# Attention and two routed expert layers on one core: code moved at both ends of the attention

## The chip, the cores and the metric

The kernel runs on one core of one Trainium2 chip. Its five instruction queues are PE (TensorE, matmuls and transposes; PEld is its weight load), DVE (VectorE), ACT (ScalarE), POOL (GpSimd) and SP (SyncE, which here only issues DMAs). The metric is the device time of one execution in microseconds (us).

## What is computed

```python
# q, k, v: (4 batches, 8 heads, 768, 64) f32; n_global = 8, n_local = 96
scores = q @ k.T / 8 - slope[h] * dist        # per batch and head
scores = where(global key or 0 <= row - col < n_local, scores, -1e9)
a = softmax(scores);  x = (a @ v) as (3072 tokens, 512)

# first expert layer: each token to the expert of its largest logit
e = argmax(x @ w_gate);  g = softmax(x @ w_gate)[e] * sigmoid(x @ w_output_gate)[e]
y = g * (relu(x @ w1[e]) @ w2[e])             # 8 experts, 512 -> 1024 -> 512
# second expert layer: greedy assignment with 384 tokens per expert
out = relu(y @ v1[e2]) @ v2[e2]
```

## The kernel before

**Attention.** 32 heads are worked as 16 pairs of heads, two pairs in each round (`two_pairs(it, ...)`): round 0 is written out, rounds 1 to 6 are a loop, and the last (`LAST`, 7) is written out again. A round has six steps t, each for two row tiles s of 128 queries. With these inputs only a band of 256 keys is needed for a row tile, and the kernel has a function for that form on each engine (`pe_banded`, `dve_banded`, `act_banded`, `pool_banded`) and one for the general form (`..._dense`). `by_form` chooses at run time: it reads a flag, and each engine goes into an If that holds its banded function or into the Else that holds its dense one. The Else stands behind the If in the instruction stream, and what comes after both stands behind the Else.

In a step, PE computes scores (`score`, L478), turns a tile of q and k of a later pair (`turn`, L461, bank `ps_t`), turns the output columns of two steps earlier (`turn_back`, L518), turns the probabilities (`turn_probs`, L491) and multiplies by v (`value`, L509, bank `ps_o[:, 0]`). DVE adds the bias (L688), makes the low parts of q and k (`low_qk`, L662 to L670; q and k are held as a high and a low part, and scores take three products), copies turned probabilities (L699) and divides by the sums (`norm`, L717). ACT does the exponentials (L820), the high parts (`high_qk`, L798 to L804), the other half of the copies (L829), and copies the output columns from PSUM to `o_cols` (`copy_cols`, L836). The bias table is made once on DVE (`dve_far`, L561 to L592), ahead of the low parts of pair 0. `turn` of a pair waits for its loads (`qk_in`); from pair 1 on it also waits until the low parts have been read out of `ps_t` (`qk_kept`).

**Loads and stores.** SP issues, in this order: pairs 0 and 1 of k, q and v, the gate weights, a 2 MB broadcast of the second gate, then q and k of pair 2. After that, for each pair in turn: q and k of the pair after the next but one once `qk_turned` allows it, v two pairs ahead once `valued` allows it, and the six stores of x once `normed` allows them. The first weights (`raw`, L2108) are issued behind the last stores.

**Logits and routing.** Behind the If and Else, `pe_logits` waits for all norms, turns the 24 tiles of x (L943, four banks in rotation), and multiplies each group of two tiles by the gates (`group_logits`, L970); ACT and DVE make high and low parts (L985, L1004), and in the last eight tiles also the first expert's w1 (L990, L1011). `dve_routing1` is one chain of small operations that sorts the tokens into blocks; PE helps with ranks (L1061) and a table (`pe_table`, L1075). From the table DVE makes the row numbers (`rows_i`, L1167), POOL copies one column of them (L1557) and gathers the first block's 128 rows of x (L1560) into `xg`. ACT meanwhile converts w2 and `wg_all` (L1228, L1231), then makes an exponential that the gates need (L1234).

**First block.** `keep_busy(18)` gives PE 18 matmuls of 512 columns on zeros (L1067), whose result nobody reads; then come `turn_x(0)` (L1261), `up(0)` (L1275), `turn_x(1)`, a second table (L1075), `turn_h(0)` (L1286), and from there blocks of 24 plus 24 matmuls (L1275, L1298) in a loop. DVE's part of that start is `low_x(0)`, the gate table, the low part of w2, `low_x(1)`, and then `dve_gates` (L1213), which waits for PE's second table.

## Time and profile before

| | us |
|---|---|
| median of 3 runs | 1052.54 |
| lowest and highest | 1049.64, 1052.82 |
| the profiled execution | 1050.72 |
| its span in the trace | 1049.0 |
| attention (first work to last norm) | 0 to 213 |
| logits, routing, start of the first block | 213 to 283 |
| blocks of the first expert layer | 283 to 632 |
| end of that layer, second routing, second layer | 632 to 1049 |

The profile gives each instruction's start and duration from the span's start, and for an engine's idle time what ended it. "issue" stands for idle time that ended with nothing the profile shows. PEclk is the clock granted to TensorE as a share of 2.4 GHz; it has two levels, 1.00 and 0.50, and values between them are averages over a stretch. Times in the rows below are of the profiled execution.

### The profile page before, as it was taken

Reading aid. Unit: us, or ns where it says so; the run is one execution under the profiler, and the core shown is the slowest. Engines: PE = TensorE matmul, PEld = TensorE weight load, DVE = VectorE, ACT = ScalarE, POOL = GpSimd, SP = SyncE. Lnnn points to the kernel's source line nnn. Section 1 sums busy time; section 2 is a strip of 40 time slices with the busy share of each in tenths; the row PEclk is TensorE's granted clock in tenths of the full one; section 3 lists DMA queues with packets and bytes.
Section 4 is the critical chain, followed back from the end, with each engine's and each line's share of the span. In section 5 each row is a group of like instructions: output and inputs, shape, how many; then the busy total and the mean of one; then the engine's idle time right before and its main releaser. Section 6 shows DMA issues by size and latency. Waiting matters only on the chain.

```text
span 1049.0 us, 22340 instructions
## 1 busy us (share of the span) xinstructions
PE 919.3 (88%) x6394; PEld 773.8 (74%) x6397; DVE 680.0 (65%) x1823; ACT 451.2 (43%) x982; POOL 191.1 (18%) x247
## 2 busy tenths in 40 slices
PE   6889999884999999999999985444599999999994
PEld 4767777773788888888888873333398989899993
DVE  4778888758766968869877784555554645463521
ACT  3778888746344352535525350000042524343410
POOL 1222322300111111111111110000203212321211
PEclk8899999987899999999999996555699999999998
DMA  9577677342351524515334251000135353635100
GB/s 213 110 160 169 161 172 165 85 178 81 111 201 41 209 69 171 200 50 200 121 129 150 93 190 57 2 2 2 34 108 209 123 198 133 220 115 203 42 31 31
DMA packets 146567, 129.40 MB, mean 123 GB/s; under 512 B 102464, under 2 KB 114752, under 8 KB 146368
## 3 DMA queue, kind: packets, MB, share of 16 engines
q1 hardware_dynamic: 137696, 99.68, 31.8%
q0 software_dynamic: 8800, 28.84, 8.1%
q8 instruction: 35, 0.57, 0.2%
q14 instruction: 36, 0.29, 0.1%
HBM read 107.79 MB, written 20.71 MB: 122 GB/s over the span
## 4 chain that ended last, share of the span: by engine, by line
PE 72%; DVE 9%; issue 6%; SPq 5%; DMA 3%; DVEq 2%; ACT 1%; POOL 0%; ACTq 0%; POOLq 0%
PE ps_o L1298 14%; PE ps_s L1275 14%; PE ps_o L1640 9%; PE ps_s L1624 6%; PE ps_pT L1624 6%; PE ps_s L1640 4%; PE ps_t L1801 3%; DMA qn<-in_q 2%; PE ps_pT L1286 2%; PE ps_o L509 2%; SPq L2053 2%; SPq L2072 1%; PE ps_t L461 1%; PE ps_t L1261 1%; PE ps_s L478 1%
## 5 line engine op out<-in xcount | busy, mean ns | idle before, releaser
L1298 PE MATMUL ps_o<-w_split_parts,hs 128*128 x696 | 169.2, 399 | 6.3 <-issue 6.3
L1275 PE MATMUL ps_s<-w_split_parts,xs 128*128 x696 | 165.8, 394 | 1.1 <-ACT xs L1367 1.1
L1298 PEld LDWEIGHTS ps_o<-w_split_parts,hs 128*128 128x128 f32 x696 | 130.1, 190 | 33.9 <-issue 7.1
L1485 DVE SCALAR_TENSOR_TENSOR product<-y_sb,wg_all 128x512 bf16<-128x512 f32 x224 | 145.8, 689 | 11.4 <-issue 6.7
L1275 PEld LDWEIGHTS ps_s<-w_split_parts,xs 128*128 128x128 f32 x696 | 128.9, 189 | 26.6 <-issue 1.3
L820 ACT ACTIVATE arena_p<-arena_p,min_s 128x256 f32<-128x256 f32 (+1 forms) x192 | 92.3, 484 | 29.6 <-DVE min_s L688 28.8
L1640 PE MATMUL ps_o<-w_split_parts,hs 128*128 128x512 f32 x384 | 94.1, 397 | 0.0
L1476 DVE TENSOR_TENSOR w_split_parts<-raw,w_split_parts 128x1024 f32 (+1 forms) x68 | 78.7, 1221 | 20.3 <-ACT w_split_parts L1386 19.0
L1640 PEld LDWEIGHTS ps_o<-w_split_parts,hs 128*128 128x128 f32 x384 | 70.2, 188 | 15.9 <-ACT hs L1674 2.9
L1720 DVE TENSOR_TENSOR w_split_parts<-raw,w_split_parts 128x1024 fp32r<-128x1024 f32 x56 | 68.6, 1225 | 18.7 <-ACT w_split_parts L1682 18.5
L1375 ACT ACTIVATE hs<-ps_pT 128x512 fp32r<-128x512 f32 x58 | 31.7, 597 | 113.1 <-PE ps_pT L1286 113.1
L1667 ACT ACTIVATE xs<-ps_t 128x512 fp32r<-128x512 f32 x22 | 13.2, 599 | 142.0 <-PE ps_t L1611 141.8
L1624 PE MATMUL ps_s<-xs,w_split_parts 128*128 128x384 f32 x384 | 69.6, 335 | 1.5 <-issue 1.5
L688 DVE CUSTOM_DVE_ANT_0 arena_p<-ps_s,arena_b 128x256 f32<-128x256 f32 (+1 forms) x144 | 54.1, 398 | 24.0 <-PE ps_o L478 8.2
L1624 PEld LDWEIGHTS ps_s<-xs,w_split_parts 128*128 128x128 f32 x384 | 67.3, 188 | 2.8 <-issue 1.7
L1624 PE MATMUL ps_pT<-xs,w_split_parts 128*128 128x384 f32 x384 | 69.1, 334 | 0.0
L1624 PEld LDWEIGHTS ps_pT<-xs,w_split_parts 128*128 128x128 f32 x384 | 66.8, 188 | 0.0
L1674 ACT ACTIVATE hs<-ps_s 128x384 fp32r<-128x384 f32 x32 | 15.8, 493 | 117.9 <-PE ps_s L1624 117.9
L1386 ACT ACTIVATE w_split_parts<-raw 128x1024 f32 (+1 forms) x64 | 62.4, 1055 | 9.0 <-issue 7.3
L1710 DVE SCALAR_TENSOR_TENSOR hs<-ps_s,hs 128x384 fp32r<-128x384 f32 x32 | 17.7, 553 | 75.0 <-ACT hs L1674 75.0
L1682 ACT ACTIVATE w_split_parts<-raw 128x1024 fp32r<-128x1024 f32 x56 | 59.0, 1054 | 0.0
L1566 POOL DMA_DIRECT2D y_rows<-y_sb x31 | 17.9, 577 | 211.3 <-ACT y_sb L1393 206.4
(307 smaller groups left out, 1690.5 us busy)
## 6 DMA issues: line engine op xcount, KB each, us to landing
raw<-in_moe_w SPq DMA_DIRECT2D x32, 2048.0 KB, 9.2
y_rows<-y_sb POOLq DMA_DIRECT2D x31, 256.0 KB, 2.3
kn<-in_k SPq DMA_DIRECT2D x32, 192.0 KB, 3.5
qn<-in_q SPq DMA_DIRECT2D x32, 192.0 KB, 3.6
vn<-in_v SPq DMA_DIRECT2D x32, 192.0 KB, 2.9
x_rows<-arena_x SPq DMA_DIRECT2D x96, 64.0 KB, 1.6
va<-in_v SPq DMA_DIRECT2D x32, 120.0 KB, 2.7
wg_rows<-in_moe_w_gate SPq DMA_DIRECT2D x1, 2048.0 KB, 7.6
```

The costliest lines, as they stand in the source:

```text
L688: nc.vector.tensor_tensor_reduce(out=neg_b[:, s % STEPS_HELD, hh, 0:w], in0=SCORE_BANKS[t % 2 * 2 + hh][:, side:side + w], in1=bias[:, par ...
L820: nc.scalar.activation(probs_b[:, s % STEPS_HELD, hh, 0:w], neg_b[:, s % STEPS_HELD, hh, 0:w], ACT.Exp, scale=-1.0, bias=min_s[:, slot:slo ...
L1275: last = nc.tensor.matmul(ps_s[:, f, :], xs[:, a, c * P:(c + 1) * P], weights(par, w, cols), start=(n == 0), stop=(n == len(passes) - 1))
L1298: last = nc.tensor.matmul(ps_o[:, 0, :], hs[:, a, c * P:(c + 1) * P], weights(par, 2 + w, slice(c * DM, (c + 1) * DM)), start=(n == 0), st ...
L1375: nc.scalar.activation(hs[:, 0, f * HALF:(f + 1) * HALF], ps_pT[:, f, :], ACT.Copy).then_inc(h_high, 1)
L1386: nc.scalar.activation(weights(par, 2 * kind, cols), raw[:, kind, cols], ACT.Copy).then_inc(hi_done, 1)
L1476: low = nc.vector.tensor_tensor(weights(par, 2 * kind + 1, cols), raw[:, kind, cols], as_f32(weights(par, 2 * kind, cols)), ALU.subtract)
L1485: nc.vector.scalar_tensor_tensor(product[:, e % 2, :], y_sb[:], 1.0, wg_all[:, e, :], ALU.mult, ALU.mult, accum_out=log_now[:, e:e + 1])
L1624: last = nc.tensor.matmul(HID_BANKS[f % 4], ws[:, par, w, at:at + P], xs2[:, a, c, :], start=(n == 0), stop=(n == len(passes) - 1))
L1640: last = nc.tensor.matmul(OUT_BANKS[j], hs2[:, a, c, j * P:(j + 1) * P], ws[:, par, 2 + w, f * DM:(f + 1) * DM], start=(half == 0 and n == ...
L1682: nc.scalar.activation(ws[:, 1 - par, 2 * kind, cols], raw[:, kind, cols], ACT.Copy).then_inc(hi_done, 1)
L1720: low = nc.vector.tensor_tensor(ws[:, 1 - par, 2 * kind + 1, cols], raw[:, kind, cols], as_f32(ws[:, 1 - par, 2 * kind, cols]), ALU.subtract)
```

## The change

Six edits. (1) On DVE, the low parts of pair 0 come ahead of the last part of the bias table (`low_parts()` in `dve_far`). (2) PE has ten matmuls on the constant tile `warm` (result unread) between the turns of pair 0 and `score(0, 0)`. (3) Pair 1's second turn goes to the bank `ps_o[:, 0]` and stands next to its first. (4) In the last round, `value` of step 5 writes the bank `ps_s[:, 0]` and stands ahead of `turn_back` of step 4; `o_cols` has two halves; `value` waits once for both tiles' probabilities. (5) Logits and routing, and DVE's start of the experts, go inside both branches of `by_form`; in the banded branch the first three tiles wait for the first batch's norms alone, the fourth for all, and the rotation of banks is another. ACT's last exponential (`act_gates`) and everything after it stay behind the branches; `keep_busy` has 10 instead of 18. (6) The first gather takes its row numbers from `rows_i` itself, without POOL's copy.

```diff
--- before
+++ after
@@ -138,8 +138,8 @@
 arena_p = at("arena_p", starts[6], [P, 3 * PART_P])
-o_cols = at("o_cols", 4 * sum(sizes), [P, 2 * P])
-assert 4 * (sum(sizes) + 2 * P) <= WSPLIT // 2
+o_cols = at("o_cols", 4 * sum(sizes), [P, 2, 2 * P])
+assert 4 * (sum(sizes) + 4 * P) <= WSPLIT // 2
@@ -419,16 +419,23 @@
     two_pairs(LAST, True)
+ps_t_whole = ps_t[:]
...
-    return FIRST_TURNS[g] if isinstance(pair, int) and pair == 0 else ps_t[:]
+    if isinstance(pair, int) and (pair == 0 or pair == 1 and g == 1):
+        return FIRST_TURNS[g]
+    return ps_t_whole
...
+def out_bank(it, t):
+
+    return ps_s[:, 0, :] if isinstance(it, int) and it == LAST and t == TWOS - 1 else ps_o[:, 0, :]
@@ -440,7 +447,7 @@
             for nth, g in turns_of(first, last_one).get(t, [])[which]]
-FRONT, MORE = slice(0, 1), slice(1, None)
+FRONT, MORE = slice(0, 2), slice(2, None)
@@ -453,7 +460,7 @@
             pe.wait_ge(qk_in[par], nth * 64 + 64)
-        if not (isinstance(pair, int) and pair == 0):
+        if turn_bank(pair, g) is not FIRST_TURNS[g]:
@@ -497,16 +504,15 @@
             pe.wait_ge(v_in[par], it * 96 + 96)
-        pe.wait_ge(normed, it * 6 + t + NORM0)
+        pe.wait_ge(normed, it * 6 + t - (isinstance(it, int) and it == LAST and t == TWOS - 1) + NORM0)
+        pe.wait_ge(p_kept, it * 12 + 2 * t + 2 + ATT0)
                 for s in (2 * t, 2 * t + 1):
-
-            pe.wait_ge(p_kept, it * 12 + s + 1 + ATT0)
...
-                    last = nc.tensor.matmul(ps_o[hh * D:hh * D + D, 0, at:at + P], tiles[:, par, a:a + D],
+                    last = nc.tensor.matmul(out_bank(it, t)[hh * D:hh * D + D, at:at + P], tiles[:, par, a:a + D],
@@ -515,7 +521,7 @@
         for j in range(2):
-            last = nc.tensor.transpose(ps_o[:, 0, j * P:(j + 1) * P], o_cols[:, j * P:(j + 1) * P], ident[:])
+            last = nc.tensor.transpose(out_bank(it, t)[:, j * P:(j + 1) * P], o_cols[:, t % 2, j * P:(j + 1) * P], ident[:])
@@ -536,12 +542,14 @@
         if last_one:
+            value(it, TWOS - 1)
                     turn_back(it, TWOS - 2)
-            value(it, TWOS - 1)
...
+    for n in range(10):
+        nc.tensor.matmul(ps_pT[:, 1, :], warm[:, 0:P], warm, start=True, stop=True)
@@ -584,6 +592,7 @@
     global_far(tmp[:, P:2 * P], key[:, 0:P], tmp[:, 0:P])
+    low_parts()
@@ -711,7 +719,7 @@
         dve.wait_ge(o_turned, it * 6 + t + 1)
-        o3 = ps_o[:, 0, 0:2 * P].rearrange("p (i c) -> p i c", c=D)
+        o3 = out_bank(it, t)[:, 0:2 * P].rearrange("p (i c) -> p i c", c=D)
@@ -736,8 +744,11 @@
                 norm(it, t)
-    for g in range(3):
-        low_qk(0, 0, g)
+    def first_low():
+        for g in range(3):
+            low_qk(0, 0, g)
+
+    dve_far(dve, True, first_low)
@@ -830,10 +841,10 @@
         act.wait_ge(valued, it * 24 + 4 * t + 4 + ATT0)
-        if not (isinstance(it, int) and it == 0 and t == 0):
-
-            act.wait_ge(o_turned, it * 6 + t)
-        nc.scalar.activation(o_cols[:], ps_o[:, 0, 0:2 * P], ACT.Copy).then_inc(o_copied, 1)
+        if not (isinstance(it, int) and it == 0 and t < 2):
+
+            act.wait_ge(o_turned, it * 6 + t - 1)
+        nc.scalar.activation(o_cols[:, t % 2, :], out_bank(it, t)[:, 0:2 * P], ACT.Copy).then_inc(o_copied, 1)
@@ -905,14 +916,16 @@
     pool_attention(pool, False)
-def by_form(eng, banded, dense):
+def by_form(eng, banded, dense, then):
...
+        then(eng, True)
             with eng.Else():
                 dense(eng)
+        then(eng, False)
@@ -922,7 +935,7 @@
-TURN_BANKS = [ps_t[:], ps_o[:, 0, :], ps_o[:, 1, :], ps_s[:, 2, :]]
+TURN_BANKS = [ps_t[:], ps_o[:, 1, :], ps_s[:, 2, :], ps_o[:, 0, :]]
@@ -931,11 +944,15 @@
     return TURN_BANKS[t % 4].rearrange("p (c r) -> p c r", c=DC)
-def pe_logits(pe):
-
-    pe.wait_ge(normed, 3 * PAIRS + NORM0)
+def pe_logits(pe, ahead):
+
+    if not ahead:
+        pe.wait_ge(normed, 3 * PAIRS + NORM0)
             pe.wait_ge(consts, 8)
             for t in range(TILES):
+        if ahead and t in (0, 3):
+
+            pe.wait_ge(normed, (3 * HP if t == 0 else 3 * PAIRS) + NORM0)
@@ -1230,8 +1247,10 @@
     nc.scalar.activation(wg_all[:], wg_rows[:].rearrange("p d e -> p e d"), ACT.Copy).then_inc(wg_all_made, 1)
+def act_gates(act):
+
             act.wait_ge(r_s, 2)
-    nc.scalar.activation(m_open[:, 0:C], t2b[:, 0:C], ACT.Exp, scale=-1.0).then_inc(r_e, 1)
+    nc.scalar.activation(m_open[:, 0:TILES], t2b[:, 0:TILES], ACT.Exp, scale=-1.0).then_inc(r_e, 1)
@@ -1531,13 +1553,15 @@
             last_block(b)
-    nc.vector.memset(logits_2[:], 0.0)
-    dve.drain()
-    dve.wait_ge(wg_all_made, 1)
-    low_x(0)
-    dve_gate_table(dve)
-    low_w(0, 0, 1, range(4), n=0)
-    low_x(1)
+    if start_only:
+        nc.vector.memset(logits_2[:], 0.0)
+        dve.drain()
+        dve.wait_ge(wg_all_made, 1)
+        low_x(0)
+        dve_gate_table(dve)
+        low_w(0, 0, 1, range(4), n=0)
+        low_x(1)
+        return
@@ -1550,15 +1574,17 @@
     def gather(b):
+        rows = rows_i
...
-        nc.gpsimd.tensor_copy(row_now[:], rows_i[:, bass.ds(b, 1)]).then_inc(row_copied, 1)
-        pool.wait_ge(row_copied, b + 1)
-        apart(pool)
+            rows = row_now
+            nc.gpsimd.tensor_copy(row_now[:], rows_i[:, bass.ds(b, 1)]).then_inc(row_copied, 1)
+            pool.wait_ge(row_copied, b)
+            apart(pool)
                 nc.gpsimd.indirect_dma_start(out=xg[:], out_offset=None, in_=x_dram[:, :],
-                                     in_offset=bass.IndirectOffsetOnAxis(row_now[:, 0:1], 0),
+                                     in_offset=bass.IndirectOffsetOnAxis(rows[:, 0:1], 0),
@@ -2175,6 +2201,11 @@
     pool_experts2(pool)
+def dve_first_route(dve, is_banded):
+    dve_logits(dve)
+    dve_routing1(dve)
+    dve_expert_start(dve)
@@ -2190,21 +2221,27 @@
     nc.vector.tensor_copy(form_i[:], form_f[:, 2:3]).then_inc(form_known, 1)
-    by_form(dve, dve_banded, dve_dense)
-    dve_logits(dve)
-    dve_routing1(dve)
+    by_form(dve, dve_banded, dve_dense, dve_first_route)
...
+def act_first_route(act, is_banded):
+    act_logits(act)
+    act_routing1(act)
...
-    by_form(act, act_banded, act_dense)
-    act_logits(act)
-    act_routing1(act)
+    by_form(act, act_banded, act_dense, act_first_route)
+    act_gates(act)
...
+def pe_first_route(pe, is_banded):
+    pe_logits(pe, is_banded)
+    pe_ranks(pe, 1, TILES)
+    pe_table(pe, ps_t[:], 0, TILES, 2, BLK1)
@@ -2215,11 +2252,8 @@
     pe.wait_ge(consts, 4)
-    by_form(pe, pe_banded, pe_dense)
-    pe_logits(pe)
-    pe_ranks(pe, 1, TILES)
-    pe_table(pe, ps_t[:], 0, TILES, 2, BLK1)
-    keep_busy(18)
+    by_form(pe, pe_banded, pe_dense, pe_first_route)
+    keep_busy(10)```

On DVE, at the start of the attention (`k_low`, `q_low` are the low parts, `arena_b` the bias table), before:

```order
L572 TENSOR_TENSOR arena_p<-arena_p 128x128
L587 COPY arena_b<-arena_p 128x32
L589 TENSOR_TENSOR arena_b<-arena_b,arena_p 128x128
L592 TENSOR_SCALAR arena_b<-arena_b,slopes 128x384 x2
L662 TENSOR_TENSOR k_low<-ps_t,k_high 128x4x128
L663 TENSOR_TENSOR k_low<-ps_t,k_high 128x5x32
L666 TENSOR_TENSOR k_low<-ps_o,k_high 128x2x128
```

and now:

```order
L580 TENSOR_TENSOR arena_p<-arena_p 128x128
L670 TENSOR_TENSOR k_low<-ps_t,k_high 128x4x128
L671 TENSOR_TENSOR k_low<-ps_t,k_high 128x5x32
L674 TENSOR_TENSOR k_low<-ps_o,k_high 128x2x128
L675 SCALAR_TENSOR_TENSOR q_low<-ps_o,q_high 128x256
L678 SCALAR_TENSOR_TENSOR q_low<-ps_o,q_high 128x512
L596 COPY arena_b<-arena_p 128x32
```

The five low parts moved ahead of the last four operations on the table.

On PE, at the end of the last round (L509 is `value`, L518 `turn_back`, L912 the jump over the Else), before:

```order
L509 MATMUL ps_o<-arena_p,va 64x128 x2
L509 MATMUL ps_o<-arena_p,vn 64x128 x2
L518 MATMUL ps_o<-ident,o_cols 128x128 x2
L509 MATMUL ps_o<-arena_p,va 64x128 x2
L509 MATMUL ps_o<-arena_p,vn 64x128 x2
L509 MATMUL ps_o<-arena_p,va 64x128 x2
L509 MATMUL ps_o<-arena_p,vn 64x128 x2
L518 MATMUL ps_o<-ident,o_cols 128x128 x2
L912 UNCONDITIONAL_BRANCH
```

and now (L515 is `value`, L524 `turn_back`, L960 a tile of x, L987 the logits of two tiles):

```order
L515 MATMUL ps_o<-arena_p,vn 64x128 x2
L515 MATMUL ps_s<-arena_p,va 64x128 x2
L515 MATMUL ps_s<-arena_p,vn 64x128 x2
L515 MATMUL ps_s<-arena_p,va 64x128 x2
L515 MATMUL ps_s<-arena_p,vn 64x128 x2
L524 MATMUL ps_o<-ident,o_cols 128x128 x2
L524 MATMUL ps_s<-ident,o_cols 128x128 x2
L960 MATMUL ps_t<-ident,arena_x 128x128 x4
L960 MATMUL ps_o<-ident,arena_x 128x128 x4
L960 MATMUL ps_s<-ident,arena_x 128x128 x4
L960 MATMUL ps_o<-ident,arena_x 128x128 x4
L987 MATMUL ps_pT<-lxs,wgs 32x256 x8
```

Both values now stand ahead of both turns back, and no branch stands between them and the tiles of x.

On PE, between the table and the first block (the Else's copy of the routing stands ahead of it), before:

```order
L1075 MATMUL ps_t<-arena_t 128x62 x24
L1067 MATMUL ps_o<-product 128x512 x18
L1261 MATMUL ps_t<-ident,xg 128x128 x4
```

and now, first the end of the banded branch and then what its jump leads to, behind the Else:

```order
L1092 MATMUL ps_t<-arena_t 128x62 x24
L923 UNCONDITIONAL_BRANCH
...
L1084 MATMUL ps_o<-product 128x512 x10
L1280 MATMUL ps_t<-ident,xg 128x128 x4
```

The jump that stood behind the attention stands behind the table.

## Rows read from the trace of the kernel before

**Rows 1.** Chain that ended last; stretch: PE, PEld, DVE, ACT, POOL busy, clock, DMA.

```profile
PE 72%; DVE 9%; issue 6%; SPq 5%; DMA 3%; DVEq 2%; ACT 1%; POOL 0%; ACTq 0%; POOLq 0%
...
283.00:632.00 349.00, 343.52 (x1679) 286.09 (x1677) 271.52 (x608) 155.35 (x232) 57.34 (x84) 1.00 0.40 141
```

**Rows 2.** Timeline at the start: start, us, engine, line, operation, [idle before, releaser].

```profile
10.99 0.18 DVE L587 COPY arena_b<-arena_p 128x32 f32<-128x32 f32 x1
...
12.10 0.68 DVE L662 TENSOR_TENSOR k_low<-ps_t,k_high 128x512 fp32r<-128x512 f32 x1
...
14.34 0.47 PE L478 MATMUL ps_s<-k_high,q_high 64*128 64x128 f32 x2 [4.06 <-DVE q_low L670]
...
29.18 1.12 PE L461 MATMUL ps_t<-ident,kn 128*128 128x128 f32 x4 [3.03 <-DMA qn<-in_q]
```

**Rows 3.** Busy time and granted clock at the start of the logits, columns as in rows 1.

```profile
215.80:218.00 2.20, 2.15 (x10) 2.19 (x11) 0.40 (x1) 0.78 (x2) 0.00 (x0) 0.50 0.39 107
```

**Rows 4.** Timeline at the end of the attention.

```profile
209.14 0.38 ACT L836 ACTIVATE o_cols<-ps_o 128x256 f32<-128x256 f32 x1 [0.46 <-PE ps_o L509]
...
210.53 0.44 PE L509 MATMUL ps_o<-arena_p,va 128*64 128x128 f32 x4 [0.52 <-DVE arena_x L717]
...
212.17 0.26 ACT L979 ACTIVATE wgs<-wg 128x64 fp32r<-128x64 f32 x1
212.61 0.42 DVE L717 TENSOR_TENSOR arena_x<-ps_o,sums 128x256 f32<-128x256 f32 x1 [2.13 <-PE ps_o L518]
215.56 0.23 DVE L995 TENSOR_TENSOR wgs<-wg,wgs 128x64 fp32r<-128x64 f32 x1 [2.52 <-issue]
215.85 1.08 PE L943 MATMUL ps_t<-ident,arena_x 128*128 128x128 f32 x4 [3.27 <-issue]
```

**Rows 5.** DMA by queue and kind, 213 to 214.5 us: packets, MB, share.

```profile
q8 instruction: 1, 0.02, 5.0%
q14 instruction: 1, 0.01, 2.0%
```

**Rows 6.** Timeline of DVE and PE in the logits.

```profile
218.45 0.69 DVE L1004 TENSOR_TENSOR lxs<-ps_o,lxs 128x512 fp32r<-128x512 f32 x1 [0.16 <-ACT lxs L985]
...
224.04 0.31 PE L956 MATMUL ps_s<-ident,logT 32*128 32x32 f32 x2
...
225.23 0.60 PE L943 MATMUL ps_t<-ident,arena_x 128*128 128x128 f32 x4
...
227.40 0.60 PE L943 MATMUL ps_o<-ident,arena_x 128*128 128x128 f32 x4
```

**Rows 7.** Timeline around PE's filler matmuls and the gather.

```profile
263.04 5.10 PE L1067 MATMUL ps_o<-product 128*128 128x512 bf16 x17 [0.22 <-issue]
268.57 0.63 PE L1261 MATMUL ps_t<-ident,xg 128*128 128x128 f32 x4 [0.43 <-issue]
270.27 5.73 PE L1275 MATMUL ps_s<-w_split_parts,xs 128*128 x24 [1.07 <-ACT xs L1367]
...
263.72 0.19 POOL L1557 COPY row_now<-rows_i 128x1 int32<-128x1 int32 x1 [69.88 <-DVE rows_i L1167]
264.95 1.26 POOL L1560 DMA_INDIRECT xg<-x_rows,row_now  x1 [1.05 <-issue]
```

**Rows 8.** The gather's line: time from issue to landing.

```profile
DMA to landing us min/median/max: 3.4/5.0/6.7
```

**Rows 9.** Timeline: the two waits that the other jumps now stand ahead of.

```profile
267.38 0.22 ACT L1234 ACTIVATE arena_t<-arena_t 128x24 f32<-128x24 f32 x1 [3.79 <-DVE arena_t L1188]
...
280.57 0.19 DVE L1213 COPY gates<-ps_o 128x31 f32<-128x31 f32 x1 [2.38 <-PE ps_o L1075]
```

**Rows 10.** Timeline: matmuls at the start of the program, and PE behind the block loop.

```profile
1.86 6.61 PE L2216 MATMUL ps_o<-arena_x 128*128 128x512 bf16 x20 [1.86 <-DVE arena_x L2184]
...
631.63 0.79 PE L1298 MATMUL ps_o<-w_split_parts,hs 128*128 x1 [5.48 <-issue]
```

10 lines of the change are left out of this document (6 added, 4 removed).

## Prediction

> **What bounds the kernel now.** The page's chain of work that ended last is read first: PE holds 72% of it [rows 1]. The busy time by stretch says where that is a rule: between 283 and 632 us PE works 343.52 of 349 us at clock 1.00 [rows 1], so a block that starts earlier by so many microseconds ends the run earlier by as many. The change does not touch those blocks. What it touches is the attention's two ends and the way from there to the first block, and for these I read the timeline at each gap: what does PE wait for when it starts again, and would an earlier start of its work move that?
>
> **The start of the attention: nothing.** The bank, the ten filler matmuls and the moved low parts all lie ahead of one wait. PE turns pair 2's first tiles at 29.18 after 3.03 us without work, released by the load of q [rows 2]. SP issues that load behind everything of pairs 0 and 1 and the gate weights; no computed value stands between (it needs pair 0's turns, which PE has ended at 14.34 - 4.06 = 10.28 [rows 2]). The edits bring `score(0, 0)` forward by the part of the table that is now behind the low parts, 10.99 to 12.10, about 1.1 us [rows 2]; the ten matmuls cost nothing while they end before the score does start, and PE has 4.06 us free there [rows 2]. Twenty like them took 6.61 us at the start of the program, ten at half clock among them [rows 10]: ten take 2.1 to 4.3 us, and the larger figure would eat the 1.1 us, again ahead of the same wait. What is late next is the load at 29.18, unmoved, so the gain is 0. Bounds: 0, and -3.03 if the load did come earlier. I take 0: the row names the load. Pair 1's other bank and the joined turns end ahead of it too; `value`'s single wait for both tiles changes nothing in the rounds, since `turn_probs` ahead of it has already waited for the same copies.
>
> **The end of the attention.** Before, the last `value` starts at 210.53, after 0.52 us of waiting for the norm that frees its bank [rows 4]. The value before it has ended when ACT copies its columns, at 209.14 [rows 4]. With a bank of its own the last value follows directly, near 209.1: 1.4 us earlier. Its copy, turn and norm follow as before (to 212.61 + 0.42 = 213.03 [rows 4]), and the other step's turn and norm lie inside them, since PE and DVE are idle there. Last norm: 211.6. **-1.4 us.**
>
> **The jump.** Between the last norm (213.03) and PE's first tile (215.85) lie 2.82 us in which PE waits for nothing that is shown; its own pause is 3.27, DVE's 2.52 [rows 4]. In it stands the jump over the Else, and two instruction loads run in just this stretch [rows 5]. I read the gap as the price of the jump: 2.5 to 3.3 us. ACT has a jump there too and starts its next instruction at 212.17, at once [rows 4]; its Else is the shortest of the three. *The Trainium skill ("Runtime: NRT & Kernel Launch", Instruction fetch mechanics) says that a taken branch to a target outside the fetched window stalls until the page is loaded; the trace agrees, with loads at 213 to 214.5 and 2.5 to 3.3 us of pause. The same rule speaks against the change: the jump is not removed but moved, with a longer Else to jump over.* That is the second half of the sum.
>
> **The logits.** In the changed kernel no jump lies between. PE has ended its last turn 3.27 ahead of 215.85, at 212.58 [rows 4]; 1.4 earlier is 211.15, and tiles 0 to 2 need only norms that are long done, so they start there. Before, tile 1's low part was ready at 218.45 + 0.69 = 219.14 [rows 6], 3.29 after the first turn's start, at clock 0.50 [rows 3]. At full clock the two turns take half: a tile's turn is worth some 0.43 less, so 2.4 us: 213.6. From there PE does two tiles in 2.17 us (225.23 to 227.40 [rows 6]). Two such periods end near 217.7, where before the same point was 224.04 [rows 6]. So everything behind is about **6.4 us** earlier; in this are the 1.4 of the last value, the 2.8 of the jump, and some 2.2 of half clock and of tiles that start ahead of the norm. Bounds: -4.2 if PE went through the logits at half clock all the same, -6.9 if the first tiles hide entirely. I take -6.4, since PE no longer stands still for 3 us ahead of them. The routing is one chain on DVE and moves as a whole; its loads have been there for long.
>
> **Table to first block.** Here the jump comes back. In the old times: PE ends the table at 262.82 (0.22 ahead of 263.04), runs its fillers until 268.14, and turns the first block's rows at 268.57 [rows 7]. The gather lands at 264.95 + 3.4 = 268.35 at the earliest [rows 7, 8], so before both ended together. Now the jump comes first: 262.82 + 3.27 = 266.1. The ten fillers follow. The 17 shown took 5.10 us [rows 7], a mix of both clock levels; after a pause of 3.3 us (after which PE restarted at 0.50 in rows 3) I take the half rate. The twenty at the start show it: if some run at half clock and the rest in half the time, 6.61 us is 10 and 10 at 0.44 and 0.22 [rows 10]. Ten at half clock are 4.3 us: 270.4, against 268.57. **+1.9 us.** The gather without POOL's copy comes 0.2 (the copy) to 1.2 us (up to the issue at 264.95) earlier [rows 7]; PE is now later than it, so that is worth 0. Bounds: with DVE's pause of 2.52 and fillers at the mix of before (3.0 us) PE would be ready at 268.3, -0.2 us; with the longest pause of the trace, 5.48 [rows 10], +4.1 us. I take the middle, since it is PE's own pause at the same jump.
>
> **The other moved jumps.** ACT's now stands behind the conversion of `wg_all` and ahead of an instruction for which ACT has waited 3.79 us [rows 9]: hidden for any price up to that. DVE's stands behind `low_x(1)`, ahead of `dve_gates`, where DVE has waited 2.38 us [rows 9] against a price of 2.52: 0.1 late, and the gates are wanted only by `down_(0)`, a whole `up` later. Both 0. Who waits behind DVE's jump is ACT's `high_h(0)`, with the same slack; if the price were 5.5, `high_h(0)` would be 3.1 late, still inside the 5.73 us of an `up` [rows 7].
>
> **The sum.** -6.4 + 1.9 = -4.5 us. On the profiled execution: span 1049.0, time 1050.72, so 1046.2. The median is 1.82 above that execution: 1052.54 - 4.5 = **1048.0**.
>
> **Rivals.**
> *PE stays at half clock into the first block (20%).* If the ten fillers after the jump don't bring the clock up, `turn_x(0)` and much of `up(0)` run at half rate: of its 5.73 us [rows 7] some 2 are added. For it: half as many fillers, and a pause ahead. Against it: ten at half clock sufficed at the start of the program by the reckoning above. -4.5 + 2.0 = -2.5: **1050.0**.
> *The gap is not the jump (10%).* Then PE still stands still before the logits, and pays nothing behind the table. *The Trainium skill ("Advanced Engine Details and Errata", Control Flow Timing) gives an always-taken branch some 51 ns, by which the 2.8 us would have another cause.* What remains is the 1.4 us at the end of the attention and, behind the table, fillers that end sooner (10 at half clock from 263.04: 267.3) so that the gather, 0.2 to 1.2 earlier, decides: -0.7. Together -2.1: **1050.4**. Against it: two engines pause alike just there, and instruction loads stand in it.
> *The start counts (12%).* If pair 2's load came as much earlier as PE waits for it at most, up to 3.03 [rows 2] would be added; half of that gives -6.0: **1046.5**. Against it is the row itself, as no edit touches SP ahead of it.
> *Slower: a loop that now reloads its code (5%).* All code behind the logits moves. If the block loop's body came to lie so that its back jump needs a load in each of its 22 rounds, PE would pay up to 2.5 us for each. It decides from 4.5 / 22 = 0.2 us a round; at 2.5 it gives +50, **1103**. Against it: PE's 343.52 of 349 us [rows 1] leave 0.25 us a block for all pauses together, so the loop runs without loads now, and its body is not longer.
>
> **How the numbers follow.** Forecast 53% (1048.0), half clock in the block 20%, not the jump 10%, the start 12%, slower 5%. A measurement of this kernel tells 0.3%, 3.2 us, from no change. Faster by more: the start's 12 and most of the forecast's 53 (with the bounds of the jump its own range is -2.3 to -6.6), 49: with a few of the half clock's 20 it is 0.64. Within: 0.31. Slower: 0.05. The range takes in the forecast's bounds, the two cases near 1050 and the start's: 1045.0 to 1051.0; outside lie the reloading loop, the far half of the start's case, and a jump at 5.5 us together with the half clock.
>
> **What would show it.** Right: PE's wait for q near 29.2, unmoved; PE's first tile of x near 211.2, ahead of the last norm's end at 211.6; clock 1.00 through the logits; the table's last matmul near 256.4, then some 3.3 us of pause and ten fillers of 0.43; `turn_x(0)` near 264.1; the blocks at the old pace. Wrong: a pause of over 1 us between the last norm and group 0's logits; fillers of 0.21; an idle PE between fillers and `turn_x(0)`, which would say that the gather decides; clock 0.50 in `up(0)`; PE's wait for q at another time than 29.2. The prediction fails most easily in the second half, where the price of a jump is taken from one place to another.

## The result

The changed kernel takes 1045.53 us in the median of five runs (1045.08 to 1046.24), the kernel before 1052.54 (1049.64 to 1054.29): a ratio of 0.9939, 95% interval 0.9921 to 0.9957, or 7.0 us less. In a later series the same two kernels gave 1047.84 (9 runs, 1044.77 to 1053.83) and 1054.16 (16 runs, 1050.19 to 1058.32), ratio 0.9946, 0.9921 to 0.9971: 6.3 us less. The forecast was 1048.0, range 1045.0 to 1051.0. The profiled execution took 1046.24 us with a span of 1044.5, which is 4.5 less than the span before.

### The profile after

First the start, PE's timeline of the changed kernel (start, us, engine, line, operation, in brackets the idle time before it and what ended it), to be held against [rows 2]:

```profile
13.26 0.33 PE L485 MATMUL ps_s<-k_high,q_high 64*128 64x128 f32 x2 [0.92 <-DVE q_low L678]
...
29.40 1.11 PE L468 MATMUL ps_t<-ident,kn 128*128 128x128 f32 x4 [6.56 <-DMA qn<-in_q]
```

The first score comes 1.08 us earlier (14.34 to 13.26), and PE then waits 6.56 us instead of 3.03 for the same load, which lands at 29.40 instead of 29.18. What the start gained was waited away.

Next the end of the attention and the first tiles of the logits, to be held against [rows 4, 6]. The second piece is the granted clock of that stretch (columns: PE, PEld, DVE, ACT, POOL busy, clock, DMA share, GB/s), to be held against [rows 3]:

```profile
205.87 1.04 PE L498 MATMUL ps_pT<-ident,arena_p 128*128 128x128 f32 x8
...
209.60 0.60 PE L960 MATMUL ps_t<-ident,arena_x 128*128 128x128 f32 x4
209.80 0.42 DVE L725 TENSOR_TENSOR arena_x<-ps_s,sums 128x256 f32<-128x256 f32 x1 [0.16 <-PE ps_s L524]
...
212.30 1.08 PE L987 MATMUL ps_pT<-lxs,wgs 128*32 128x256 f32 x8 [0.79 <-DVE lxs L1021]
```

```profile
209.60:212.00 2.40, 1.91 (x18) 1.67 (x16) 1.73 (x5) 1.77 (x4) 0.00 (x0) 1.00 0.20 57
```

PE turns its first tile of x at 209.60, ahead of the last norm (209.80 to 210.22), without a pause, and at clock 1.00. The pause of 3.27 us and the half clock of [rows 3, 4] are gone. In the kernel before, the last turn of the probabilities stood at 207.00 and the first tile at 215.85, 8.85 us apart; now 3.73.

Then the way from the table to the first block, PE and POOL, against [rows 7]:

```profile
253.88 1.15 PE L1092 MATMUL ps_t<-arena_t 128*128 128x62 bf16 x8 [0.18 <-DVE arena_t L1100]
257.30 4.45 PE L1084 MATMUL ps_o<-product 128*128 128x512 bf16 x10 [2.26 <-issue]
261.54 1.06 PE L1280 MATMUL ps_t<-ident,xg 128*128 128x128 f32 x4
...
256.81 1.27 POOL L1586 DMA_INDIRECT xg<-x_rows,rows_i  x1 [63.99 <-issue]
```

```profile
257.30:261.50 4.20, 4.20 (x10) 1.56 (x11) 3.06 (x16) 0.22 (x1) 0.78 (x1) 0.50 0.24 68
263.50:269.20 5.70, 5.68 (x25) 4.68 (x26) 5.70 (x8) 0.60 (x1) 1.03 (x1) 1.00 0.17 46
277.00:626.00 349.00, 342.61 (x1676) 285.34 (x1674) 272.06 (x609) 155.91 (x233) 55.80 (x84) 1.00 0.40 140
```

```profile
q8 instruction: 1, 0.02, 1.1%
q14 instruction: 1, 0.01, 0.3%
```

The last piece is the instruction loads between 255 and 262 us (packets, MB, share), as in [rows 5]. The jump stands where it was expected, behind the table, as a pause of 2.26 us that ends with nothing the profile shows; ten fillers follow at half clock, 4.45 us; PE goes from them into the turn of the first gathered tile with no wait, so the gather does not decide. The first product runs at 1.00. The block loop is as full as in [rows 1] (342.61 of 349 us).

Last, the two other moved jumps, against [rows 9]:

```profile
259.65 0.22 ACT L1253 ACTIVATE arena_t<-arena_t 128x24 f32<-128x24 f32 x1 [3.54 <-DVE arena_t L1205]
...
275.54 0.19 DVE L1230 COPY gates<-ps_o 128x31 f32<-128x31 f32 x1 [4.42 <-issue]
276.29 1.09 ACT L1394 ACTIVATE hs<-ps_pT 128x512 fp32r<-128x512 f32 x2 [5.90 <-DVE gates L1234]
```

ACT's is hidden under its wait for DVE. DVE's shows as 4.42 us, and ACT waits behind it.

### Where 4.5 us went, and why the median says 6 to 7

One table holds all fourteen profiled executions of this study by five marks on PE. Each number is the distance of two starts in a trace: P is the last turn of the probabilities, X the first x tile of the logits, T the last group of the table's matmuls, D the first down product, U the first product of the second layer, V its second half.

| kernel | P at | P to X | X to T | T to D | D to U | U to V | V to PE's last |
|---|---|---|---|---|---|---|---|
| before | 207.00 | 8.85 | 45.84 | 26.47 | 471.20 | 4.24 | 268.68 |
| start's edits alone | 207.50 | 8.80 | 45.42 | 25.34 | 471.24 | 6.60 | 268.62 |
| attention's end alone | 206.91 | 7.18 | 44.93 | 25.59 | 471.90 | 4.26 | 268.92 |
| branch alone | 209.92 | 6.09 | 43.90 | 27.10 | 473.33 | 6.93 | 268.92 |
| no If | 207.26 | 6.09 | 43.88 | 26.93 | 473.38 | 6.71 | 268.70 |
| short Else | 209.37 | 6.08 | 44.38 | 27.26 | 473.77 | 7.02 | 268.62 |
| changed | 205.87 | 3.73 | 44.28 | 27.75 | 471.61 | 5.83 | 268.62 |
| changed, again | 207.87 | 3.72 | 43.88 | 25.94 | 472.08 | 4.25 | 268.79 |
| changed, old start | 208.77 | 3.72 | 44.78 | 26.35 | 472.19 | 5.81 | 268.70 |
| changed, 12 fillers for q | 206.88 | 3.72 | 43.83 | 27.31 | 472.15 | 5.82 | 268.81 |
| changed, 24 fillers late | 207.36 | 3.72 | 43.86 | 26.19 | 471.59 | 4.24 | 268.62 |
| changed, 2 fillers | 207.06 | 3.72 | 43.87 | 29.95 | 471.67 | 4.24 | 268.92 |
| table behind the branch | 208.95 | 3.72 | 43.85 | 26.72 | 471.45 | 4.26 | 268.63 |
| the same, 24 late | 206.22 | 3.72 | 43.86 | 26.67 | 472.14 | 4.24 | 268.66 |

Between the profiled executions of the two kernels the columns give: -1.13 in the attention, -5.12 from P to X, -1.56 from X to T, +1.28 from T to D, +0.41 to U, +1.59 from U to V, -0.06 behind it; together -4.59. Two of these terms are not the change's. P lies anywhere from 205.87 to 209.92 in these traces, also among kernels with the same attention (changed: 205.87 and 207.87). The clock goes with it: in the five traces with P at 207.87 or later it is 0.50 for longer at the start, either from the load of q until about 39 us (branch alone, table behind the branch) or once more between 55 and 60 us (short Else, changed again, old start); in the nine with P up to 207.50 neither happens. And U to V has two values, about 4.25 and 5.8 to 7.0, though no edit touches that code. It is the granted clock during that product, as these rows of the kernel before and of the changed one tell (PE only; PE busy, clock, DMA share, GB/s; then PE's timeline).

```profile
759.40:763.60 4.20, 4.20 (x24) 1.00 0.60 158
...
759.36 4.40 PE L1624 MATMUL ps_s<-xs,w_split_parts 128*128 128x384 f32 x24 [1.46 <-issue]
```

```profile
755.00:758.00 3.00, 3.00 (x12) 0.57 0.61 178
...
753.24 5.99 PE L1650 MATMUL ps_s<-xs,w_split_parts 128*128 128x384 f32 x24 [1.46 <-issue]
```

The profiled execution of the kernel before had the good value, that of the changed kernel the bad one. P to V leaves the attention's chance out, though not that of the clock behind U: 556.60 and 557.40 us for the kernel before and the one with the start's edits alone, 553.20 and 549.87 for the two executions of the changed kernel. The means are 5.5 us apart. That lies inside both intervals of the timed runs (4.5 to 8.3, and 3.1 to 8.3 us), a little below their middles.

T to D holds a piece of clock too. Ahead of the second up product PE turns hidden tiles (`turn_h(0)`); that turn and the product behind it run partly at half clock in some executions. PE's timeline of the changed kernel's two executions:

```profile
273.62 1.88 PE L1305 MATMUL ps_pT<-ident,h_sb 128*128 128x128 f32 x8
```

```profile
274.64 1.05 PE L1305 MATMUL ps_pT<-ident,h_sb 128*128 128x128 f32 x8
```

From there to D it takes 8.01 us in the first and 6.77 in the second; the kernel before has 7.80, with the start's edits alone 6.72. Up to the start of this turn the traces agree better: T to it is 18.62 to 18.85 us in the three traces with 18 fillers and the jump behind the attention, and 19.11 to 19.74 in the six with ten fillers behind the jump.

### The profile page after: what moved, and what is told of

It reads as the page before. It is cut to its first block, busy times and chain, and to the rows that moved or that the text cites. A ratio compares the mean times of both kernels' runs of the same rounds, so it can differ in the third digit from the quotient of the medians.

```text
span 1044.5 us, 22307 instructions
## 1 busy us (share of the span) xinstructions
PE 918.0 (88%) x6398; PEld 772.5 (74%) x6399; DVE 679.4 (65%) x1823; ACT 450.4 (43%) x982; POOL 188.8 (18%) x246
## 4 chain that ended last, share of the span: by engine, by line
PE 71%; DVE 9%; issue 6%; SPq 6%; DMA 3%; ACT 2%; DVEq 2%; POOL 0%; ACTq 0%; POOLq 0%
PE ps_o L1317 14%; PE ps_s L1294 14%; PE ps_o L1666 9%; PE ps_s L1650 7%; PE ps_pT L1650 6%; PE ps_s L1666 4%; DMA qn<-in_q 3%; PE ps_t L1827 3%; PE ps_pT L1305 2%; SPq L2079 2%; PE ps_o L515 2%; SPq L2098 2%; PE ps_t L1280 1%; PE ps_pT L498 1%; PE ps_t L468 1%
## 5 line engine op out<-in xcount | busy, mean ns | idle before, releaser
L1294 PE MATMUL ps_s<-w_split_parts,xs 128*128 x696 | 166.1, 394 | 0.9 <-ACT xs L1386 0.9
L1294 PEld LDWEIGHTS ps_s<-w_split_parts,xs 128*128 128x128 f32 x696 | 129.0, 189 | 26.8 <-issue 1.3
L1394 ACT ACTIVATE hs<-ps_pT 128x512 fp32r<-128x512 f32 x58 | 31.6, 596 | 114.4 <-PE ps_pT L1305 108.4
L1650 PE MATMUL ps_s<-xs,w_split_parts 128*128 128x384 f32 x384 | 71.2, 341 | 1.5 <-issue 1.5
L1650 PEld LDWEIGHTS ps_s<-xs,w_split_parts 128*128 128x128 f32 x384 | 68.9, 192 | 2.8 <-issue 1.7
L1650 PE MATMUL ps_pT<-xs,w_split_parts 128*128 128x384 f32 x384 | 69.1, 334 | 0.0
L1650 PEld LDWEIGHTS ps_pT<-xs,w_split_parts 128*128 128x128 f32 x384 | 66.8, 188 | 0.0
```

Of the source, the lines that this page charges most:

```text
L1294: last = nc.tensor.matmul(ps_s[:, f, :], xs[:, a, c * P:(c + 1) * P], weights(par, w, cols), start=(n == 0), stop=(n == len(passes) - 1))
L1394: nc.scalar.activation(hs[:, 0, f * HALF:(f + 1) * HALF], ps_pT[:, f, :], ACT.Copy).then_inc(h_high, 1)
L1650: last = nc.tensor.matmul(HID_BANKS[f % 4], ws[:, par, w, at:at + P], xs2[:, a, c, :], start=(n == 0), stop=(n == len(passes) - 1))
```

## The experiments

### Each part alone, in the kernel before

The first series (before: 1052.95, 35 runs, 1049.42 to 1057.77) put each group of edits alone into the kernel before. First the start: low parts ahead of the table, the second bank, the ten fillers.

```
-            dve_far(dve, True)
...
+            def first_low():
+                for g in range(3):
+                    low_qk(0, 0, g)
+            dve_far(dve, True, first_low)
...
+            for n in range(10):
+                nc.tensor.matmul(ps_pT[:, 1, :], warm[:, 0:P], warm, start=True, stop=True)
             score(0, 0)
```

> The kernel before with the edits at the start of the attention alone (low parts ahead of the last of the bias table, pair 1's second turn in a bank of its own, ten matmuls on the constant tile). Theory 1 (the load decides): pair 1's scores run some 3 us earlier, PE waits about 6.5 us for the load of q instead of 3.0, starts again at 29.2 to 29.4 as before, and every mark behind it and the total stay within 0.5 us of before. Rival (the start counts): the marks behind 29.4 come earlier, 0.7 us at the turn near 55 and 1.1 us at the end of the attention, as they do in the changed kernel, and the total is 1 us or more lower.

It took 1053.41 us (12 runs, 1050.31 to 1055.98), ratio 1.000, 0.9984 to 1.0015. Its PE timeline at the start:

```profile
13.04 0.33 PE L482 MATMUL ps_s<-k_high,q_high 64*128 64x128 f32 x2 [0.75 <-DVE q_low L676]
...
29.10 1.12 PE L465 MATMUL ps_t<-ident,kn 128*128 128x128 f32 x4 [7.54 <-DMA qn<-in_q]
```

The score is 1.3 us earlier than in [rows 2] and the wait for q 4.5 us longer; q lands at 29.10. The start counts nothing, as the wait's releaser had said.

Then the attention's end: a bank of its own for the last value, and two places for the columns.

```
+        def out_bank(it, t):
+            return ps_s[:, 0, :] if isinstance(it, int) and it == LAST and t == TWOS - 1 else ps_o[:, 0, :]
...
-                    turn_back(it, TWOS - 2)
                     value(it, TWOS - 1)
+                    turn_back(it, TWOS - 2)
```

> The kernel before with the edits of the last round alone (second bank for the last value, halves of o_cols, one wait for both tiles' probabilities in value). Theory 1: the last norm ends 1.4 to 1.7 us earlier against the turned probabilities of step 5, nothing changes in the rounds before, and the total is 1.4 to 1.7 us lower. Rival (value's single wait shortens the rounds): the turn near 181 us also comes about 1 us earlier, and the total is 2.5 us or more lower.

It took 1050.1 us (11 runs, 1047.34 to 1054.81), ratio 0.9975, 0.9957 to 0.9993: 2.6 us less, with 0.7 to 4.5 inside the interval. In the table above P to X is 7.18 against 8.85: 1.67 us from the last value. Timeline of PE and DVE:

```profile
208.58 0.39 PE L512 MATMUL ps_o<-arena_p,vn 128*64 128x128 f32 x4
208.80 0.39 PE L512 MATMUL ps_s<-arena_p,va 128*64 128x128 f32 x4
...
210.83 0.42 DVE L720 TENSOR_TENSOR arena_x<-ps_s,sums 128x256 f32<-128x256 f32 x1 [0.15 <-PE ps_s L521]
```

The two values stand back to back (ps_o, then ps_s), and the last norm ends at 211.25, 4.34 us behind P where it was 6.03. The rest of the 2.6 is X to T, 0.9 us shorter (the first turn of x took 0.71 us instead of 1.08, so less of the start ran at half clock). The total of 2.6 would also fit the rival of this expectation, but the mark that it names doesn't move: the turn near 181 us starts at 181.40, before at 181.39. So `value`'s single wait does not shorten the rounds.

Then logits and routing inside the branch, with ten fillers, but without the early tiles:

```
             with eng.If(is_banded > 0):
                 banded(eng)
+                then(eng, True)
             with eng.Else():
                 dense(eng)
+                then(eng, False)
...
-            keep_busy(18)
+            keep_busy(10)
```

> The kernel before with logits and routing inside the branches alone, all tiles waiting for all norms, ten fillers behind the table. Theory 1 (a jump costs 2.3 to 3.3 us wherever it stands): PE's first tile follows the last norm within 0.3 us and runs at clock 1.00, 2.7 us of pause and about 1.9 us of half clock are gone, and 1.0 to 1.9 us come back behind the table: total -2.7 to -3.7 us. Rival (the pause is not the jump): PE still stands still near 2.8 us behind the last norm, and the total is within 1 us of before.

It took 1050.33 us (12 runs, 1049.31 to 1054.93), ratio 0.9983, 0.9968 to 0.9999: 1.8 us less by the ratio, 0.1 to 3.4 inside the interval, where 2.7 to 3.7 were expected. PE's timeline at the two places:

```profile
216.01 0.66 PE L945 MATMUL ps_t<-ident,arena_x 128*128 128x128 f32 x4 [0.52 <-DVE arena_x L717]
...
263.72 4.05 PE L1069 MATMUL ps_o<-product 128*128 128x512 bf16 x9 [2.67 <-issue]
```

The pause ahead of the logits is gone; PE waits 0.52 us for the norm, and P to X is 2.76 us shorter. It comes back behind the table with 2.67 us. This execution's attention ended 2.9 us late (209.92 against 207.00). PE's busy time and clock near its start:

```profile
37.00:39.00 2.00, 2.00 (x11) 0.50 0.00 0
39.00:41.00 2.00, 2.00 (x29) 0.98 0.00 0
```

PE runs at half clock until 39 us behind the load of q, where in the kernel before the clock was coming back from 33 us on (0.88 between 33 and 35 us): none of the edits is at work there. D to U is 2.1 us longer than before (473.33), 1.8 of it between the end of the block loop and the last logits. There DVE pauses 5.11 us instead of 3.72 with no releaser shown, ACT waits for DVE, and PE for ACT, 3.48 us instead of 0.78.

### Is the gap the jump, and is it the distance?

The gap of 2.82 us was read as the price of a jump over the Else. The first test takes the If out altogether, and leaves out the dense form, which these inputs do not use:

```
-            with eng.If(is_banded > 0):
-                banded(eng)
-            with eng.Else():
-                dense(eng)
+            banded(eng)
```

> The kernel before without the If and Else over the form: the banded functions stand straight in the program, the dense ones are left out, nothing else is changed (18 fillers). Theory 1 (the pause is the jump): PE's first tile follows the last norm within 0.3 us, DVE's pause of 2.5 us goes too, logits at clock 1.00, and nothing comes back behind the table: total -4.3 to -5.0 us. Rival (another cause, such as waits for the gates or the constants): the pause of 2.8 us stays and the total is within 1 us of before.

It took 1054.17 us (12 runs, 1050.98 to 1056.94), ratio 1.0008, 0.999 to 1.0026: no gain at all, where 4.3 to 5.0 us were expected, though its PE timeline shows the gap gone. Timeline of DVE and PE behind the block loop:

```profile
646.00 0.18 DVE L1924 TENSOR_SCALAR arena_t<-used 128x31 f32<-128x31 f32 x1 [1.59 <-issue]
...
757.54 6.87 PE L1620 MATMUL ps_s<-xs,w_split_parts 128*128 128x384 f32 x24 [1.46 <-issue]
```

P to X is 6.09, as in the kernel with the branch edits, and D stands 4.0 us earlier than before (288.16 to 284.16). Then 2.2 us are lost from D to U. About half of it stands in the first row: DVE pauses 1.59 us for nothing that is shown, in the second routing, where the kernel before had no such pause, and the routing is 1.1 us longer. The other 1.1 us lie ahead of U, where PE waits 2.27 us for the gathered rows of the second layer instead of 1.27. Another 2.5 us are the half clock of U to V.

The second test keeps the If and empties only its other side:

```
             with eng.Else():
-                dense(eng)
+                eng.wait_ge(consts, 3)
```

> The kernel before with the If kept, but its other side (the dense form, which does not run on these inputs) left out: one wait that is already met stands in its place, so the jump behind the attention goes over one instruction instead of some 240 on TensorE. Theory 1, the 3.27 us pause at 215.85 is the reading of instructions from a place far off: the pause is gone as in the kernel without the If (its first x tile came at 213.35, 0.52 us of wait for the norm), the first x tile stands 0.9 to 1.3 us behind the last turn back, and the table ends 3 to 4.5 us earlier than 262.8. Theory 2, the branch itself and its being resolved cost the 2.8 us, whatever the distance: the pause stays above 2.5 us. In the time of the whole either may be drowned, since the kernel without the If gained 4.0 us by 284 us and gave 4.7 back behind 632 us (VectorE waited 1.59 us for no semaphore at 646.00 where it had not, the gathered rows landed 1.0 us later, the first product of the second layer took 6.87 us instead of 4.40): 1048.5 to 1054 us.

Its series had the kernel before at 1051.73 (29 runs, 1049.41 to 1058.0). It took 1052.41 us (12 runs, 1050.44 to 1056.02), ratio 1.0002, 0.9984 to 1.0019. Its PE timeline, and one row of DVE:

```profile
215.45 0.66 PE L943 MATMUL ps_t<-ident,arena_x 128*128 128x128 f32 x4 [0.52 <-DVE arena_x L717]
...
260.80 6.19 PE L1067 MATMUL ps_o<-product 128*128 128x512 bf16 x18
...
648.37 0.41 DVE L1923 TENSOR_REDUCE span<-logits 128x1 f32<-128x248 f32 x1 [5.25 <-issue]
```

The branch is there and costs nothing: P to X is 6.08 us, to 0.01 the value without any If, and 2.77 less than before. The instruction loads fit: before, two of them stand in the gap [rows 5]; here none falls between 212 and 216 us, and none between 208 and 214 in the kernel without the If. So the 2.8 us are the price of jumping far, not of branching. How far is too far no run here tells: tried were one instruction, the whole dense form, and in the changed kernel the dense form with a second copy of the routing, which cost no more (2.26 to 3.18 us of pause). The 240 instructions that the expectation names for the dense form are too few: in `pe_dense` a round has 24 steps of 14 matmuls, and a round is written out twice. *The Trainium skill ("Runtime: NRT & Kernel Launch", Instruction fetch mechanics) says of a taken branch whose target lies outside the fetched window that it stalls for a load; this pair of runs agrees, 2.8 us with the dense form in between and 0 without. The 51 ns that the Trainium skill ("Advanced Engine Details and Errata", Control Flow Timing) gives for an always-taken branch does not price the far one.*

But again the whole did not gain, and again D to U is longer (473.77 against 471.20). DVE's pause ahead of the second routing took 2.76 us in the kernel before and 5.25 here, which is 2.5 of these 2.6 us; another 2.8 are the half clock of U to V. Both kernels without the dense code show such a pause, at different places. The code behind the If moved in both, and I take the pauses for instruction loads that fall otherwise: five such loads stand in the pause of 5.25 us, one in that of 1.59, and one in the 2.76 us of before. By itself that cause was not tested.

### Is it the start, or the clock?

The next series ran the changed kernel once more beside three variants of it (before: 1054.16).

> The changed kernel unchanged, timed in the same rounds as the next three, so that they have something to be held against. Theory A: the profiled execution of the kernel before was a favourable one. Its first product of the second layer ran at granted clock 1.00 in 4.40 us (759.36), where the changed kernel needed 5.99 us and three of the four partial kernels 6.76 to 7.09 us, so the 4.5 us between the two spans are too few and the median gains 6.5 to 8 us: ratio 0.992 to 0.994. Theory B: the spans tell the size, and the 7.0 us between the medians of five runs each are chance: ratio 0.995 to 0.997.

1047.84 us (9 runs), ratio 0.9946, 0.9921 to 0.9971. In its profile U to V took 4.25 us and the span was 1043.3, 5.7 below the one before. The interval allows both theories of this expectation; the table of marks speaks for the first, since the 4.25 came without any edit.

With the start put back as it was, and all else changed:

```
-            def first_low():
-                for g in range(3):
-                    low_qk(0, 0, g)
-            dve_far(dve, True, first_low)
+            for g in range(3):
+                low_qk(0, 0, g)
...
-            for n in range(10):
-                nc.tensor.matmul(ps_pT[:, 1, :], warm[:, 0:P], warm, start=True, stop=True)
             score(0, 0)
```

> The changed kernel with its start put back as in the kernel before (low parts of the first pair behind the table of biases, one turn bank, no ten fillers), all else changed. Theory 1: the start counts nothing, since the turn that waits for the load of q ends its wait at 29.18 us before and at 29.40 after: within 0.5 us of the changed kernel, and the x tiles of the logits start where they did, at 209 to 210 us. Theory 2: the 1.1 us by which the last turn of the probabilities came earlier (207.00 to 205.87) is the start's: 1.1 us slower than the changed kernel, and its last turn of the probabilities is at 207.0 again. Theory 3: the start edits keep TensorE's clock from falling late in some executions (in the kernel with the branch edits alone it was 0.50 until about 39 us instead of 33, and the attention ran 2.9 us late): the median is 1 to 3 us slower and the runs spread over more than 4 us instead of the 1.2 us of the changed kernel.

1047.54 us (8 runs, 1045.06 to 1051.09), ratio 0.9934, 0.991 to 0.9957: the same as the changed kernel, within 0.3 us, and its runs spread no wider (6.0 us against 9.1), so the third theory falls too; the late clock until 39 us also came once with the start's edits in place (table behind the branch, below). From both sides the start counts nothing. The 1.13 us by which P came earlier in the first profile were chance: with the same edits it stands at 207.87 in the second. Of the 1.13, 0.7 are there at the next turn that waits for a load: it starts at 54.40 in that profile, at 55.11 before and 55.01 in the second.

If the wait for q lets the clock fall, fillers in it should help:

```
                         score(it, t + 1)
+                    if first and t == 1:
+                        pe.wait_ge(p_kept, 2 + ATT0)
+                        for n in range(12):
+                            nc.tensor.matmul(ps_pT[:, 1, :], warm[:, 0:P], warm, start=True, stop=True)
```

> The changed kernel with twelve matmuls more (128x512, into a bank that is free) ahead of the turn that waits 6.56 us for the load of q until 29.40 us; the granted clock is 0.50 there from about 22 to 33 us. At half clock the twelve take about 5.2 us (0.43 us each, from the ten of 4.45 us behind the table), so they end before the load lands. Theory 1, the clock is what makes the first 10 us behind the load slow: the clock at 29 to 33 us is 1.00, the turn of kn takes 0.66 us instead of 1.11, the turn at 41.73 us comes 1.5 to 3 us earlier, and so does the end. Theory 2, VectorE or the loads set the pace behind 29.40: the clock is 1.00 and nothing at 41.73 or behind it moves by more than 0.3 us. Theory 3, the fillers are too many: the load's turn itself comes later than 29.4 by what they overrun.

1047.32 us (6 runs, 1043.72 to 1048.81), ratio 0.993, 0.9904 to 0.9956. PE's timeline, then PE busy and clock by stretch:

```profile
22.75 3.00 PE L534 MATMUL ps_pT<-arena_x 128*128 128x512 bf16 x11 [0.33 <-issue]
29.46 0.66 PE L468 MATMUL ps_t<-ident,kn 128*128 128x128 f32 x4 [3.70 <-DMA qn<-in_q]
```

```profile
26.00:29.00 3.00, 0.00 (x0) 1.00 0.78 158
29.00:31.00 2.00, 1.54 (x12) 0.88 1.13 255
31.00:33.00 2.00, 2.00 (x16) 0.50 0.64 112
```

The fillers did bring the clock up and the first turn takes 0.66 instead of 1.11 us, but they ended 3.7 us ahead of the load, and the clock fell to 0.50 at 31 us all the same. The turn that stood at 41.73 stands at 41.24, and at 41.39 in the other execution of the changed kernel. No gain that can be told; the third theory is out, the first is not refuted, since the cover had a hole. But little would come of it: PE waits for the next load in any case, here 2.82 us until 55.50.

And more fillers ahead of the second layer:

```
-            keep_busy(16)
+            keep_busy(24)
```

> The changed kernel with 24 instead of 16 fillers behind the table of the second routing, ahead of the first gathered tile of the second layer (748.50 us), whose first product took 5.99 us at clock 0.57 in 755 to 758 us. Theory 1, the pauses of PE ahead of it (1.19 and 1.46 us) let the clock fall, and fuller cover helps: the product takes 4.3 to 4.4 us; the eight fillers cost up to 0.5 us; 1 to 1.6 us faster than the changed kernel. Theory 2, when the clock falls there isn't set by these eight: it stays 5 to 7 us, and the kernel is the same or, if the fillers run at half clock (0.43 us each) and push the first gathered tile back, up to 2 us slower.

1046.48 us (6 runs, 1044.03 to 1049.92), ratio 0.993, 0.9904 to 0.9955. In its profile:

```profile
752.72 4.40 PE L1650 MATMUL ps_s<-xs,w_split_parts 128*128 128x384 f32 x24 [1.47 <-issue]
```

Full clock. With 24 fillers both traces (this and the last of the study) show it; with 16, three of the six of the changed kernel and its variants do not (5.8 us), nor do four of the six from the kernel before's side (6.6 to 7.0). That fits the first theory, but two traces are few (with five good ones in twelve, two in a row come by chance one time in six), and 1.4 us of median lie within the spread of runs. What the longer fillers do change is the pause ahead of the gathered rows: with 16 fillers PE waits about 1.2 us or more for them, with 24 it does not wait. The pause of 1.47 us ahead of the product stays.

### What the fillers and the place of the jump are worth

The last series (before: 1051.73) took the fillers behind the table from ten to two:

```
-            keep_busy(10)
+            keep_busy(2)
```

> The changed kernel with two instead of ten fillers between the table and the first gathered tile (257.30 to 261.54 us, ten at half clock, 4.45 us). Two take 0.9 us, so the turn of the first gathered tile waits for the gather instead (issued 256.81 us, landing 3.3 to 4 us later: 260.4 to 260.8). Theory 1, the fillers pay by the clock: without them the first up products run at 0.50 (the 24 matmuls of an up take 4.3 to 4.4 us at 1.00 and would take 8.7), the turn is 0.9 us earlier but the first down starts 2 to 4 us later than 281.6: slower by 2 to 4 us. Theory 2, the fillers are in the way: the clock rises in the first up all the same and the kernel is 0.5 to 1 us faster.

1050.16 us (12 runs, 1047.88 to 1054.02), ratio 0.9979, 0.9959 to 0.9999.

```profile
257.58 1.27 POOL L1586 DMA_INDIRECT xg<-x_rows,rows_i  x1 [63.59 <-issue]
...
258.07 1.04 PE L1084 MATMUL ps_o<-product 128*128 128x512 bf16 x2 [2.27 <-issue]
261.65 1.09 PE L1280 MATMUL ps_t<-ident,xg 128*128 128x128 f32 x4 [2.55 <-issue]
263.66 8.37 PE L1294 MATMUL ps_s<-w_split_parts,xs 128*128 x24 [0.93 <-ACT xs L1386]
```

PE reaches the gathered tile early and waits 2.55 us for it (the gather was issued at 257.58, 4.07 us ahead). The first up product then takes 8.37 us instead of 5.74, and T to D 29.95 instead of 25.9 to 27.8. The fillers are worth 2 to 4 us by these marks; the ratio is 0.0033 to 0.004 above those of the changed kernel, 3.5 to 4.2 us. Theory 1 holds.

Then the table's matmuls behind the branch, so that PE's jump lies ahead of its 6.85 us of waiting for DVE, and twelve fillers:

```
             pe_ranks(pe, 1, TILES)
-            pe_table(pe, ps_t[:], 0, TILES, 2, BLK1)
...
             by_form(pe, pe_banded, pe_dense, pe_first_route)
-            keep_busy(10)
+            pe_table(pe, ps_t[:], 0, TILES, 2, BLK1)
+            keep_busy(12)
```

> The changed kernel with TensorE's part of the table written behind the branch instead of inside it, and twelve fillers instead of ten: its jump now lies ahead of the table, where it waits 6.85 us for VectorE (until 251.26 us). Theory 1, a jump costs nothing where its engine waits longer than it anyway: no pause without a semaphore behind the table (2.26 us in the changed kernel), the fillers start within 0.3 us of the table's end at 255.0 us and end at 260.2 to 260.6 us, the first gathered tile is turned at about 260.7 us when its gather lands, 0.7 to 1.0 us earlier than 261.54: 0.5 to 1 us faster. Theory 2, the pause is of the code that comes next and not of the jump: it stays 2 to 3 us behind the table and the kernel is 0.9 us slower by two fillers more.

1046.78 us (10 runs, 1045.15 to 1048.8), ratio 0.9945, 0.9926 to 0.9965.

```profile
253.91 1.16 PE L1092 MATMUL ps_t<-arena_t 128*128 128x62 bf16 x8 [6.85 <-DVE arena_t L1100]
...
256.52 1.17 PE L1092 MATMUL ps_t<-arena_t 128*128 128x62 bf16 x8 [0.16 <-DVE arena_t L1100]
257.51 4.41 PE L1084 MATMUL ps_o<-product 128*128 128x512 bf16 x12
263.33 0.63 PE L1280 MATMUL ps_t<-ident,xg 128*128 128x128 f32 x4 [1.41 <-issue]
```

The pause of the jump is gone: it lies in the wait of 6.85 us, which has not grown. The fillers follow the table at once and end near 261.9; then PE waits for the gather. From the table to the first gathered turn it is 6.81 us instead of 7.66, as expected. The gain reaches `turn_h(0)`, 18.69 us behind T against 19.11 to 19.74 with ten fillers behind the jump. But T to D is 26.72, inside the 25.9 to 27.8 of the changed kernel and its variants, since that turn and the product behind it ran partly at half clock again (8.03 us to D).

Last, these edits and the fillers ahead of the second layer together:

```
-            pe_table(pe, ps_t[:], 0, TILES, 2, BLK1)
...
-            keep_busy(10)
+            pe_table(pe, ps_t[:], 0, TILES, 2, BLK1)
+            keep_busy(12)
...
-            keep_busy(16)
+            keep_busy(24)
```

> The kernel of the run before this one with 24 fillers instead of 16 behind the second table as well, which had given 1.36 us less in the median than the changed kernel in the same rounds (1046.48 against 1047.84), within what the runs spread. Both together: 1 to 2.5 us faster than the changed kernel, ratio to the kernel before 0.990 to 0.993; if the first product of the second layer needs 6 us all the same in the profile, the eight fillers do nothing and the median is that of the run before this one.

1046.19 us (8 runs, 1043.73 to 1047.95), ratio 0.9935, 0.9913 to 0.9958. Its profiled execution has the lowest span of the study, 1042.3 (as has the one with 24 fillers alone), and no half clock at U. Against the changed kernel's 0.9939 and 0.9946 that is 0.4 to 1.2 us, where 1 to 2.5 were expected, and no difference that can be told.

## Why the prediction was right, point by point

**The start, 0: right.** The row that named the load of q decided; shown from both sides.

**The end of the attention, -1.4: right in kind, -1.67 in size.** Alone, the edit took 1.67 us out of P to X. The step dated the last value by ACT's copy of the one before it (209.14). It does not wait for even that: in the second experiment it stands 0.22 us behind the group before it (208.58, 208.80), and ACT's copy follows at 209.04. That is the missing quarter of a microsecond.

**The jump, -2.8: right.** It took 2.76 us out of P to X with the branch edits, 2.76 without the If, 2.77 with a short Else.

**The logits, -6.4: right by the whole, -6.68.** P to T went from 54.69 to 48.01 us. The parts: 1.67, 2.76, 0.69 of early tiles (8.85 - 3.73 - 4.43), and 1.56 from X to T, where the half clock is gone. The forecast had the last two as 2.2; they are 2.25.

**Table to first block, +1.9: the mis-sized term.** It was added up from 3.27 us of pause and 4.3 of fillers, and forecast for the turn of the first gathered tile. From T to that turn it is 6.88 us before and 7.66 in the changed kernel: +0.8. Over the six traces with ten fillers behind the jump (7.38 to 7.88) against the three with the old arrangement (6.88 to 7.09) the mean is +0.7, and it is +0.7 again at `turn_h(0)`. Both parts were too long. The pause took 2.26 here, and 2.27, 2.66, 2.67, 2.72, 2.94 and 3.18 in the other traces with PE's jump behind the table, all less than 3.27. And ten fillers ran at half clock to their end only here (4.24 us from their start to the turn); in the other five traces the clock rose before, and they took 3.28 to 3.84. T to D itself grew by 1.28 us in the profiled pair and shrank by 0.53 in the second trace, but there the half clock at `turn_h(0)` comes and goes.

**The other jumps, 0: right for the end, too small for DVE.** The prediction took 2.52 against a wait of 2.38, 0.1 late. DVE's pause was 4.42 here and 4.67 to 5.11 in three variants; in the other five traces with the moved jump the gates wait for PE instead (2.3 to 2.7 us), so there the jump is hidden. The prediction had reckoned that even 5.5 stays under an up product, and it does: D does not wait for it.

**The sum.** -4.5 was forecast and -4.5 is the difference of the spans, but that agreement is partly luck. The change's own part is -5.40 (P to D) in that pair, chance adds -1.13 in the attention, and +1.59 of clock and +0.41 from D to U take back. With the terms as the runs give them the sum would have been -6.68 + 0.7 = -6.0 us, or 1046.6 on the median, where 1045.53 was measured. So the miss of 2.5 us is 1.5 from the terms, 1.2 of it from the +1.9, and 1.0 that the spread of the runs covers.

**The rivals.** The half clock in the first block (1050.0) did not reach the first up product with ten fillers (5.74 us at 1.00), only the turn ahead of it (1.06 us against 0.63). With two fillers it came, and cost 3.5 to 4.2 us instead of the 2.0 of the prediction; that the median of 1050.16 met the rival's 1050.0 is luck, since the forecast to which the 2.0 were added was 2.5 us too slow. "Not the jump" is refuted by the short Else. "The start counts" came nearest in number (1046.5) and is refuted as a mechanism. The slower one, a block loop that reloads, didn't occur: PE works 342.61 of 349 us, and from D to the end of the block loop it is 337.97 to 338.02 us in all fourteen traces.

## What to carry to other kernels

Ask of a jump not whether it is there but how far it goes and what its engine waits for next: 2.8 us cost nothing under a wait of 6.85 us, and nothing when the Else was short. Judge an edit by the distance between two marks around it in several traces, not by one span: the distance P to X repeats to 0.01 us (3.72 or 3.73 in all eight traces of the changed kernel and its variants) where whole runs of one kernel spread over up to 9 us. And when code is removed, look at the pauses without a releaser in all that follows: two kernels here won 2.8 us at the place, lost 2.2 and 2.6 us behind the block loop, and gained nothing in the whole.

## What the runs showed of the hardware

A far jump cost PE 2.8 us behind the attention, and showed as a pause of 2.26 to 3.18 us behind the table; with one instruction to jump over it cost nothing, and under a longer wait neither. Pauses with no releaser shown differ in the same way between layouts and executions: PE's at the end of the block loop takes 5.12 to 7.63 us in these fourteen traces (5.48 before, 6.80 in the changed kernel), DVE's ahead of the second routing 2.72 to 3.13 and once 5.25. Without the dense form DVE had a pause of 1.59 us at a place that had none. And the granted clock divides executions of one kernel: the first product of the second layer takes 4.25 us or 5.8 to 7.0, and behind the load of q half clock lasts until 32 to 35 us in twelve traces and until 39 in two, and in those two P stood at 209.92 and 208.95 against 207.00 before.

What stays open: whether the pauses that the kernels without the dense code show are instruction loads that fall otherwise, and whether the half clock of U to V came to both by chance; why DVE pauses longer behind the block loop with the branch edits alone; and whether the 24 fillers keep the clock up or were lucky twice.
